# Windowed attention on float32 operands, two heads on halves of the array, in a fused attention and gated-layer kernel; stores moved on the SP queue

## The reference, cut to what matters

```python
def _attn_ref(q, k, v):                      # 4 batches, 8 heads, 576 positions, 64 wide
    scores = scale * np.matmul(q, k.transpose(0, 1, 3, 2))
    bias = slopes[:, None, None] * (-np.abs(rel).astype(np.float32))[None, :, :]
    mask = (rel >= 0) & (rel < 128)
    scores = np.where(mask, scores + bias[None], -1000000000.0)
    scores = scores - np.max(scores, axis=-1, keepdims=True)
    attn = np.exp(scores)
    attn = attn / (np.sum(attn, axis=-1, keepdims=True) + 1e-09)
    return np.matmul(attn, v).astype(np.float32)

x = attn_out as 2304 tokens of 512
x = (1 / (1 + np.exp(-(x @ w_gate))) * (x @ w_val)) @ w_out      # 512 -> 1536 -> 512
x = (((x @ w1) * (x @ w2)) @ w3) @ moe2_w_out                    # 512 -> 1024 -> 1024 -> 512
```

## Time and profile before

| | |
|---|---|
| three timed runs | 1035.70, 1037.02, 1039.22 us; median 1037.02 |
| profiled execution | 1036.08 us, of which the profile's span is 1034.2 us |
| PE busy | 932.4 us (90%), PEld (its weight loads) 867.3 us |
| POOL, ACT, DVE busy | 736.5, 562.4 and 559.1 us |
| mean granted TensorE clock | 0.957 of full |

### The profile page before, as it was taken

How to read it: one execution, slowest core, us unless ns; L and a number is a source line. 1 busy time by engine, 2 the same in 40 slices (tenths; PEclk the granted TensorE clock), 3 DMA queues, 4 the chain that set the end, 5 groups by cost and what they waited for, 6 DMA issues and landing times. The chain is left out here.

```text
span 1034.2 us, 16072 instructions
## 1 busy us (share of the span) xinstructions
PE 932.4 (90%) x5352; PEld 867.3 (84%) x5352; DVE 559.1 (54%) x1280; ACT 562.4 (54%) x1295; POOL 736.5 (71%) x627
## 2 busy tenths in 40 slices
PE   3988787999997989977999998879987999998998
PEld 2766677999996879976999997869887999997998
DVE  5435353566655556644656655545653755555554
ACT  5867675666674644455666764555443433444340
POOL 4756988777865877758778785788745977658950
PEclk9989898999998989988999999889988999999999
DMA  6335132322121211142221221212103222202201
GB/s 221 113 100 166 45 95 79 98 88 97 48 81 36 69 58 62 51 145 78 82 71 58 87 77 48 86 47 79 62 1 123 68 76 86 78 21 82 82 22 61
DMA packets 46049, 80.79 MB, mean 78 GB/s; under 512 B 4112, under 2 KB 27280, under 8 KB 45968
## 3 DMA queue, kind: packets, MB, share of 16 engines
q1 hardware_dynamic: 45968, 79.77, 23.5%
HBM read 72.94 MB, written 6.82 MB: 77 GB/s over the span
## 5 line engine op out<-in xcount | busy, mean ns | idle before, releaser
L595 PE MATMUL quad_ps<-xs_hi,wq_hi 128*128 128x384 f32 x840 | 299.3, 356 | 23.7 <-ACT sig L866 12.1
L597 PE MATMUL quad_ps<-xs_hi,wq_lo 128*128 128x384 f32 x840 | 289.4, 344 | 0.0
L596 PE MATMUL quad_ps<-xs_lo,wq_hi 128*128 128x384 f32 x840 | 289.2, 344 | 0.0
L595 PEld LDWEIGHTS quad_ps<-xs_hi,wq_hi 128*128 128x128 f32 x840 | 164.4, 196 | 33.1 <-issue 17.0
L595 PE MATMUL o_ps<-h_hi,wo_hi 128*128 128x384 f32 x480 | 168.1, 350 | 11.3 <-DVE xf L1098 10.8
L596 PEld LDWEIGHTS quad_ps<-xs_lo,wq_hi 128*128 128x128 f32 x840 | 164.7, 196 | 0.0
L597 PEld LDWEIGHTS quad_ps<-xs_hi,wq_lo 128*128 128x128 f32 x840 | 163.8, 195 | 0.0
L597 PE MATMUL o_ps<-h_hi,wo_lo 128*128 128x384 f32 x480 | 163.3, 340 | 0.0
L596 PE MATMUL o_ps<-h_lo,wo_hi 128*128 128x384 f32 x480 | 163.0, 340 | 0.0
L1315 POOL TENSOR_TENSOR wq_lo<-wsum,wq_hi 128x1024 fp32r<-128x1024 f32 x60 | 143.7, 2396 | 7.7
L1308 POOL TENSOR_TENSOR wq_lo<-raw_q,wq_hi 128x768 fp32r<-128x768 f32 x60 | 110.8, 1846 | 53.6 <-ACT wq_hi L839 53.6
(11 more groups left out here) (89 smaller groups left out, 1811.0 us busy)
## 6 DMA issues: line engine op xcount, KB each, us to landing
raw_q<-w SPq DMA_DIRECT2D x24, 512.0 KB, 3.5
raw_q<-w_gate SPq DMA_DIRECT2D x18, 512.0 KB, 3.4
raw_q<-w_val SPq DMA_DIRECT2D x18, 512.0 KB, 4.6
wo_lo_raw<-w_out SPq DMA_DIRECT2D x18, 512.0 KB, 3.5
wo_lo_raw<-w_times_wout SPq DMA_DIRECT2D x12, 512.0 KB, 3.6
w_raw<-w3t SPq DMA_DIRECT2D x16, 256.0 KB, 3.4
q_lo_raw<-qT SPq DMA_DIRECT2D x16, 192.0 KB, 3.8
bias<-bias SPq DMA_DIRECT2D x12, 256.0 KB, 4.1
```

Of the source, the lines that this page charges most:

```text
L595: pe.matmul(out, lh, rh, start=start, stop=False, skip_group_check=onto)
L596: pe.matmul(out, lh, rl, start=False, stop=False, skip_group_check=onto)
L597: return pe.matmul(out, ll, rh, start=False, stop=stop, skip_group_check=onto)
```

## The change

- **Operands.** `q_sb`, `k_sb`, `v_sb` are loaded and used as float32; all high and low parts of q, k, v and of the turned weights are gone, and with them `keys_hi/lo`, `queries_hi/lo`, `values_hi/lo` on ACT and POOL. `scores` waits for the DMAs. There are three sets of tiles throughout, and a job's loads are issued two jobs ahead.
- **scores.** Two float32 matmuls (one a head, still on row halves) in place of six.
- **pv.** For each block of keys and head one float32 matmul of 128 rows, 64 columns of values and 128 columns of weights, whose result goes to one half of the columns of the array (two or four matmuls a step in place of three or six). `out_copy` is one instruction of 128 partitions.
- **turned.** One copy on DVE (`turned_copy`) in place of ACT's cast and DVE's subtraction.
- **The head's slots.** `scores(s)`, `turn(s-3)`, `pv(s-4)` in slot s; folds start in slot 3, and from fold 50 on there are three in a slot; 33 slots in place of 37. POOL makes all low parts of w3. DVE now runs `reciprocals(s-1)` ahead of `score(s)`. The first loads stand in another order, three memsets fewer ahead of them.
- **Stores.** The output of a pass is stored in four DMAs: two in its last section (`pair1`), two in the next pass's first section behind the loads. `out_copy` of third 2 waits only for the part that it overwrites.

```diff
-LAG_QK, LAG_SCORE, LAG_NORM, LAG_TURN, LAG_PV = 3, 4, 5, 6, 8
+LAG_NORM, LAG_TURN, LAG_PV = 1, 3, 4
...
-    return 5 + k // 2
+    return 3 + k // 2 if k < 50 else 28 + (k - 50) // 3
...
-            def store_pass(p):
-
-                sp.wait_ge(acc_done, tiles_to((p + 1) * GP - 1))
-                sp.dma_start(out_v[:, :, p * TP:(p + 1) * TP],
-                             xf[:, :].rearrange("p (o t) -> p o t", o=KB)[:, :, p % 2 * TP:(p % 2 + 1) * TP]
-                             ).then_inc(out_stored, 16)
+            def store_part(p, o):
+
+                last = tiles_to((p + 1) * GP - 1) - 8
+                sp.wait_ge(acc_done, last + 1 + max(k for k, (_, part) in enumerate(O_TILES) if part == o))
+                start = o * 2 * TP + p % 2 * TP
+                sp.dma_start(out_v[:, o, p * TP:(p + 1) * TP], xf[:, start:start + TP]).then_inc(out_stored[o], 16)
...
                 if kind == "gate":
-                    if g and g % GP == 0:
-                        store_pass(g // GP - 1)
                     if g + 1 < NG:
                         load_quad(g + 1, 0)
                     load_out(g)
...
+                if kind == "pair1" and g % GP == GP - 1 and g + 1 < NG:
+                    store_part(g // GP, 0)
+                    store_part(g // GP, 1)
+                if kind == "gate" and g and g % GP == 0:
+                    store_part(g // GP - 1, 2)
+                    store_part(g // GP - 1, 3)
...
-                sides = ((q_hi, k_hi), (q_hi, k_lo), (q_lo, k_hi))
-                for t, (left, right) in enumerate(sides):
-                    for h in range(2):
-                        rows = slice(h * D, (h + 1) * D)
-                        mm = pe.matmul(score_bank(n, h)[:, keys], left[st][rows, q], right[st][rows, where],
-                                       start=t == 0, stop=t == 2)
+                for h in range(2):
+                    rows = slice(h * D, (h + 1) * D)
+                    mm = pe.matmul(score_bank(n, h)[:, keys], q_sb[st][rows, q], k_sb[st][rows, where],
+                                   start=True, stop=True)
...
                 for c in chunks_of(n):
                     rows = slice(0, rows_of(n) if c == 1 else P)
-                    vc = slice(key_chunk(n, c) * P, (key_chunk(n, c) + 1) * P)
-                    pc = slice(c * 2 * P, (c + 1) * 2 * P)
-                    mm = product(pv_bank(n)[:, 0:2 * P], (v_hi[st][rows, vc], v_lo[st][rows, vc]),
-                                 (pt_hi[buf][rows, pc], pt_lo[buf][rows, pc]),
-                                 start=c == chunks_of(n)[0], stop=c == 1)
+                    for h in range(2):
+                        left = key_chunk(n, c) * P + h * D
+                        right = (c * 2 + h) * P
+                        mm = pe.matmul(pv_bank(n)[h * D:(h + 1) * D, 0:P], v_sb[st][rows, left:left + D],
+                                       pt[n % 2][rows, right:right + P], start=c == chunks_of(n)[0], stop=c == 1)
...
-            def turned_lo(n):
+            def turned_copy(n):
 
                 cols = pt_cols(n)
-                dve.wait_ge(pt_hi_done, n + 1)
-                nc.vector.tensor_tensor(out=cols(pt_lo[pt_of(n)]), in0=cols(turn_bank(n)), in1=cols(pt_hi[pt_of(n)]),
-                                        op=ALU.subtract).then_inc(pt_split, 1)
+                dve.wait_ge(turned, n + 1)
+                wait(dve, pv_done, n - 1)
+                nc.vector.tensor_copy(cols(pt[n % 2]), cols(turn_bank(n))).then_inc(pt_done, 1)
...
-            for s in range(SLOTS):
-                if 0 <= s - LAG_SCORE < HEAD:
-                    score(s - LAG_SCORE)
-                if 0 <= s - LAG_NORM < HEAD:
-                    reciprocals(s - LAG_NORM)
-                if 0 <= s - LAG_TURN - 1 < HEAD:
-                    turned_lo(s - LAG_TURN - 1)
+            for s in range(SLOTS + 1):
+                if 0 <= s - LAG_TURN < HEAD:
+                    turned_copy(s - LAG_TURN)
...
+                if 0 <= s - LAG_NORM < HEAD:
+                    reciprocals(s - LAG_NORM)
+                if s < HEAD:
+                    score(s)
```

More of the change, by code:

```diff
@@ L278, in build @@
         soft = [sb(ctx, f"soft{b}", [P, 2 * KW], F32) for b in range(3)]
-        pt_hi = [sb(ctx, "pt_hi0", [P, 4 * P], F32R)]
-        pt_lo = [sb(ctx, "pt_lo0", [P, 4 * P], F32R)]
+        pt = [sb(ctx, f"pt{b}", [P, 4 * P], F32) for b in range(2)]
         negmax = sb(ctx, "negmax", [P, 4], F32)
@@ L292, in build @@
             fold_sb = sb(one, "fold_sb", [P, DM], F32)
-            pt_hi.append(sb(one, "pt_hi1", [P, 4 * P], F32R))
-            pt_lo.append(sb(one, "pt_lo1", [P, 4 * P], F32R))
+            w3_raw = [sb(one, f"w3_raw{k}", [P, IB * P // 2], F32) for k in range(3)]
         h_hi = [sb(ctx, f"h_hi{b}", [P, 4 * TH], F32R) for b in range(2)]
@@ L339, in build @@
         h_hi_done, h_split = sem("h_hi_done"), sem("h_split")
-        o_done, acc_done, out_stored = sem("o_done"), sem("acc_done"), sem("out_stored")
+        o_done, acc_done, out_stored = sem("o_done"), sem("acc_done"), [sem(f"out_stored{o}") for o in range(KB)]
         def score_bank(n, h):
@@ L547, in _ @@
             for s in range(SLOTS):
-                for j in range(3, HEAD_JOBS + 1):
-                    if s == FIRST[j - 2] + LAG_QK:
+                for j in range(3, HEAD_JOBS + 2):
+                    if s == FIRST[j - 2]:
                         load_k(j)
@@ L586, in _ @@
                 sp.dma_start(out_v[:, o, start:start + TH], xf[:, acc_cols(len(PROJECTS) - 1, k)]
-                             ).then_inc(out_stored, 16)
-            sp.wait_ge(out_stored, 16 * (NPASS - 1 + 8))
+                             ).then_inc(out_stored[o], 16)
+            for o in range(KB):
+                sp.wait_ge(out_stored[o], 16 * (NPASS - 1 + 2))
         @block.tensor
@@ L626, in turn @@
                 if n < HEAD:
-                    wait(pe, pt_split, n - 1)
+                    wait(pe, pt_done, n - 1)
                 else:
@@ L807, in exponentials @@
                                      ACT.Identity, bias=tiny[0:rows, 0:1]).then_inc(sum_done, 1)
-            def turned_hi(n):
-                act.wait_ge(turned, n + 1)
-                wait(act, pv_done, n - 1 if n < HEAD else n)
-                cols = pt_cols(n)
-                nc.scalar.copy(cols(pt_hi[pt_of(n)]), cols(turn_bank(n))).then_inc(pt_hi_done, 1)
             def out_copy(n):
                 act.wait_ge(pv_done, n + 1)
-                if n >= STEPS_TO[2]:
-                    act.wait_ge(out_stored, 16)
-                rows = rows_of(n)
-                for h in range(2):
-                    op = nc.scalar.copy(out_cols(n, h), pv_bank(n)[h * D:(h + 1) * D, h * P:h * P + rows])
-                op.then_inc(x_ready, 1)
+                if n >= STEPS_TO[2] and n in UNIT_FIRST:
+                    act.wait_ge(out_stored[unit_of(n) % HP], 16)
+                nc.scalar.copy(out_cols(n), pv_bank(n)[:, 0:rows_of(n)]).then_inc(x_ready, 1)
             def x_hi(inst, j):
@@ L1322, in out_lo @@
                                         op=ALU.subtract).then_inc(wo_split, 1)
-            def splits(sec):
-                for j in range(HEAD_JOBS + 1, len(JOBS)):
-                    if sec + 1 == section_of(j):
-                        keys_lo(j)
-                        queries_lo(j)
-                for j in range(HEAD_JOBS, len(JOBS)):
-                    if sec == section_of(j):
-                        values_lo(j)
             for b in range(3):
@@ L1339, in _ @@
                     normalise(s - LAG_NORM)
-                for j in range(HEAD_JOBS + 1):
-                    if s == FIRST[j] + 1:
-                        keys_lo(j)
-                    if s == FIRST[j] + 2:
-                        queries_lo(j)
-                    if j < HEAD_JOBS and s == FIRST[j] + 6:
-                        values_lo(j)
-                if s in W3_LO_SLOT and W3_LO_SLOT[s] % 2 == 0:
+                if s in W3_LO_SLOT:
                     hf = W3_LO_SLOT[s]
@@ L1382, in _ @@
                     weight_sums(g + 1, 1)
-                    splits(sec)
                     out_lo(g)
```

224 lines of the change are left out of this document (64 added, 160 removed).

## The result

| | before | with the change |
|---|---|---|
| timed runs, median (us) | 1036.5 (1035.7 to 1039.2) | 963.9 (961.9 to 965.4) |
| ratio, 95% interval | | 0.929 (0.927 to 0.932) |
| profiled execution, its span | 1036.1, 1034.2 | 961.9, 959.6 |
| first product of pass 0 starts at | 134.5 | 118.4 |

The kernel is 7.1% faster, 72.6 us. The prediction had the sign but not the size: 1018, and 992 to 1048 as its range. What became of its terms can be read in a few rows.

What follows compares the result with a forecast made beforehand. PE was taken to bound the kernel. Against 1036.1 us, passes 26 - 40 = -14 and head 14 - 18.6 = -4.6 gave 1017.5, and with 0.9 for the median 1018; range 992 to 1048.

Steps and rivals of the forecast that it cites:

- PE's price: Float32 scores and pv cost PE about +0.5 us a step: +26 us in the passes, +14 in the head.
- I take six, the middle of four and eight: Rounds of the array for both heads' float32 matmuls; scores of 256 keys cost PE 1.08 us against 0.75.
- Rival 1: Both heads' float32 matmuls fully side by side, four rounds: +20 us in place of +40, 998 us; chance 0.15.
- The changeover: Going over to halves of the array and back costs PE 0.39 us in scores, and now in pv too.
- The waits of scores: In the passes, PE's waits in scores for POOL's low part of k go: -20.5 us.
- the six waits: PE's four large waits of scores and its waits at the starts of passes 1 and 2.
- The store: At the starts of passes 1 and 2 ACT's load no longer stands behind the store: -10.5 us.
- The clock: PE's 27.45 us of work at half clock behind the six waits costs half of it: -13.7 us.
- I give 5 back: In the passes, 5 us returned for DVE and ACT chains that come next in line at the same places.
- Priced at nothing: ACT's high parts and second copy, DVE's subtraction, stores and POOL's additional w3 work: no term in the sum.
- The head: First fold earlier -3.9 us, waits after it -9.7, half clock -5: in all -18.6, without PE's price.
- Rivals 2 and 3: Eight rounds in all 80 steps, 1058 us, chance 0.20; a third of the 58.6 saved returns as waits, 1038, chance 0.15.

Runs made afterwards that it cites:

- pv_by_head: The changed kernel with pv written head by head, head 0's matmuls for both blocks of keys and then head 1's: 966.7 us, ratio 0.934.
- parts_waited: As parts_kept, and PE's scores and pv of a job's first step in the passes also wait for POOL's subtractions: 998.4 us, ratio 0.963.
- parts_kept: The changed kernel with ACT's and POOL's work on parts of k, q and v back in the passes, PE not waiting for it: 971.0 us, ratio 0.937.
- store_back: The changed kernel with the store of a third as before, one 1.5 MB DMA ahead of the loads in passes 1 and 2: 977.3 us, ratio 0.943.
- turned_kept: The changed kernel with ACT's copy of the turned weights back in the passes, ahead of DVE's copy: 970.3 us, ratio 0.936.
- w3_first: The changed kernel with POOL's low part of w3 ahead of normalise in the head's slots: 953.2 us, ratio 0.919.
- scores_twice: The changed kernel with the two float32 matmuls of scores issued twice in the 52 steps of the passes: 978.4 us, ratio 0.945.

## Why the prediction was wrong, point by point

Forecast were -18.6 us against the profiled execution, measured -74.2. Some 37 of the difference are PE's price (+40 forecast, +2.8 measured: +5.7 in the passes, -2.9 in the head), some 19 the terms beside it (-58.6 forecast, -77.5 measured: -64.3 in the passes, -13.2 in the head).

**PE's price of the float32 step: wrong, and the largest miss.** The step that failed is "I take six, the middle of four and eight". Rival 1 had it: four rounds. The prediction's reason against it, that head 1's matmul stands whole behind head 0's, fell twice: in the trace of after, where the two start 6 ns apart, and in pv_by_head, where even four records of one head ahead cost nothing. The price itself was in the earlier trace rows: pairs at 0.12 a round, and four of these are 0.48, near the 0.43 that was measured. The changeover was right: 0.83 less the pair's 0.43 leaves 0.40 for scores, and pv has 0.79 less 0.44, or 0.35, where 0.39 was taken.

Four rounds are not the whole of it, for rival 1 itself priced them at +0.25 a step, +20 in all, and +2.8 was measured. Two more things were wrong. First, the price of pv before was read from one form, two blocks of 128 keys, at 0.73. A block of 64 keys behind one of 128 cost 1.09 then and costs 0.94 now, and scores of 128 keys went from 0.68 to 0.62, where the prediction had +0.1. Second, in the head the work of attention stands together, scores, pv, transposes. A step of 256 keys there takes, from its first start to the next fold, 0.63 + 0.59 + 0.41 = 1.63 us where it took 0.55 + 0.82 + 0.38 = 1.75. The new pv takes 0.59 there and 0.79 among whole matmuls in the passes, so that it pays nearly no changeover of its own, where the old one took 0.82 and 0.74. So it is +5.7 in place of +26 in the passes and -2.9 in place of +14 in the head.

**The waits of scores: right in place and price.** Forecast -20.5 of idle time and, of the clock behind the six waits, 9.1 that stood behind these four; parts_waited against parts_kept gives -17.3 and -11.0. (One reading is off: the weights' parts were done at 471.87, 1.6 us after the wait began at 470.30, and not 1.9.)

**The store: right.** Forecast -10.5 and a share of the clock; +8.8 idle and +6.8 clock come back with store_back.

**The clock: right mechanism, wrong extent.** The prediction priced only the stretches right behind the six waits, -13.7. It was -23.5 in the passes. The other eight stretches there, 16 us lost, stood behind waits of 1.9 to 4.0 us that the prediction left alone, for `xf`, `negmax` and `s`; three such are left, 6.2 us lost. The others went as their waits got shorter or vanished, as this one of PE for `xf` at the end of the first layer, before and with the change:

```profile
319.58 0.41 PE L595 MATMUL o_ps<-h_hi,wo_hi 128*128 128x384 f32 x1 [3.48 <-DVE xf L1098]
```
```profile
293.54 0.41 PE L571 MATMUL o_ps<-h_hi,wo_hi 128*128 128x384 f32 x1 [1.50 <-DVE xf L1007]
```

The store put back brings 6.8 us of the clock's loss, the parts 1.5, their waits another 11.0, the turned copy 5.1. Working out a clock term from the waits that a change removes leaves out the waits that it shortens.

**"I give 5 back": wrong in sign.** The same places have DVE and ACT chains, the prediction says, that the change leaves alone. It left them alone in the code, but not in time: ACT and POOL had less to do. parts_kept shows +5.8 of idle time for work that PE does not wait for, turned_kept +2.6. Forecast were 31 us of waits less these 5; the idle time of the passes fell by 40.8, near 31 + 8.4.

**"Priced at nothing": wrong by 7 and 6 us.** ACT's parts and its second copy were said to lie beside PE's work; POOL's parts had no term but the waits. parts_kept (+7.1) and turned_kept (+6.4) are what they cost, the idle time of the point above included. The cover holds inside a group of sections, and fails at the ends of layers and the start of a pass, where PE stands behind the chains of these engines: in parts_kept its wait for `xf` at the end of the first layer is 2.41 us in place of 1.50, and one for `s` early in pass 1 3.59 in place of 1.64.

**The head: too small.** Forecast -18.6 without PE's price, measured -13.2. The first fold starts at 14.9, where 13.6 was taken, and the waits after it fell from 12.7 us to 8.1, where 3 was taken; 7.2 of them are for the low part of w3. The prediction said "POOL's additional w3 work fits in the room that it gains". It does fit by its sum, but it stood behind `normalise` in the slot, and w3_first shows that this order was the cost.

**Rivals 2 and 3** did not come about. Rival 1 had the mechanism, at a chance of 0.15, but not the size: its own 998 lies inside the range and 34 us above what was measured, some 17 of it PE's price as above and 19 the terms beside it. The sign was right for the reason given, waits and half clock that go; the price that was set against them was nearly absent.

## What to carry to other kernels

A float32 matmul costs about four rounds of the array, and two of them on separate halves cost no more than one as long as all have one shape (0.43 us for 256 columns in each case): a middle between two cases is a case of its own and needs its own evidence. Taking work off engines that are "hidden" still pays where a dense engine stands behind their chains, here at the ends of layers and passes, and the larger waits mostly cost a half-clock stretch too (all three over 3 us that the change leaves in the passes do; one of 3.32 in parts_kept does not). Look in the waits that remain for an instruction that merely stands ahead of the one waited for.

## What the runs showed of the hardware

- A float32 matmul is two records with two weight loads. A pair on two row halves costs 0.43 us for 256 columns and 0.23 for 128 (scores_twice), one on two column halves 0.22 for 128 (pv of two blocks against one, 0.79 less 0.57).
- Two heads' matmuls on column halves overlap fully even if one head's four records stand ahead of the other's (0.59 us in both orders), but not across a change from 128 to 64 rows (1.44 against 0.73 us). The Trainium skill, "TensorE: Matmul & The Clock Gate", section "Part 3: Packing small matmuls", has matmuls of different tiles overlap but start in order. In the written order of pv_by_head head 1 would start behind head 0's fourth record, 0.38 us after its first, and the whole would take some 0.97 us (an estimate from the starts in its trace, 0.16, 0.11 and 0.11 apart, and 0.59 for four records of one half). It took 0.59, with the second record 13 ns behind the first, so that here the halves seem to be served apart. Which record belongs to which head the trace does not say.
- A whole float32 matmul on 128 rows and columns costs 0.43 us for 256 columns, so that among matmuls of the whole array two of them (0.89) lose little to the halves with their changeovers (0.79), and one wins (0.43 against 0.57).
- pv of two blocks on column halves takes 0.59 us from its first start to the next work, whether scores on row halves or whole matmuls stand ahead of it; a whole pv takes 0.97 behind scores and 0.70 behind whole matmuls.
- The same subtraction of 128 x 768 on DVE takes 0.96 us at 293.89 of the changed kernel and 2.55 at 301.62. POOL works beside both. At 293.89 DVE started 0.05 us ahead of POOL's instruction; at 301.62 POOL's had started at 300.84 and ended at 303.35, and DVE ended 0.82 us later. In all seven places of the changed kernel where POOL's was under way first, DVE ends 0.81 to 0.82 us behind it: these two do not run side by side but one after the other, and most of the 2.55 us is DVE waiting for POOL.
